# Expert attention scores from rounded and low parts instead of full fp32

## Chip, cores and metric

The kernel runs on one core of a Trainium2 chip. The metric is device time in microseconds (us) of one execution. PE is TensorE, DVE is VectorE, ACT is ScalarE, POOL is GpSimd, PSUM the memory that PE writes.

## What is computed

Three layers follow one another for 4 batches of 576 tokens with 512 features: windowed attention, a gated two-matrix layer, and a mixture of 4 attention experts of width 64 with the best 2 of 4 weighted by a gate. Only the experts matter here:

```python
logits = x @ w_gate
for e in range(E):                      # 4 experts
    q, k, v = x @ wq[e], x @ wk[e], x @ wv[e]          # 576 x 64 each
    scores = scale * (q @ k.transpose(0, 2, 1))
    scores = np.where(causal, -1000000000.0, scores)
    a = np.exp(scores - scores.max(-1, keepdims=True))
    a /= a.sum(-1, keepdims=True) + 1e-09
    ye = a @ v @ wo[e]
    ...                                 # added where e is one of the two chosen
```

## The kernel before

Everything is written out by hand, engine by engine, with semaphores between the engines. The same program runs for the 4 batches; in the first three, the windowed attention of the next batch is worked on beside the dense layer of this one.

**Rounded and low parts.** Most matrix products take operands split in two: `hi` is the value rounded to the type `f32r` (the profile prints it as f32 or fp32r), `lo` is the rest. `pe_passes` (lines 509 to 513) multiplies them in three passes, hi·hi, hi·lo and lo·hi, into one PSUM bank. The scores of the experts do not: `pe_scores` (line 602) multiplies whole fp32 numbers of the tensor `c_kq`, and the profile shows each such matmul as two records.

**The experts' part of a batch** (`pe_experts`, line 692). PE makes 13 projections in the order of the list `PROJECTIONS`: kq 0 to 3 (keys and queries of the first pair of experts, halves of 288 tokens; 0 and 1 are keys, 2 and 3 queries), v 0 to 4 (values and gate logits), kq 4 to 7 (the second pair). They alternate between the two banks of the PSUM tensor `MM`. ACT copies each out (`act_projection`, line 868; the queries are scaled on the way), and its semaphore `mm_out` frees the bank for the projection two further on.

Scores come in 10 tiles, the list `TILES`: for each pair, query tiles of 128 tokens against all keys up to them, so 512, 384, 256 or 128 columns, and the last 64 queries against 576. In this order: 512, 384, 576, 256, 128 columns for the first pair; 512, 576, 384, 256, 128 for the second. The two experts of a pair lie on partitions 0 to 63 and 64 to 127; the matmuls of one use the upper half of PE's rows and those of the other the lower half. For the last tile each expert also has its own half of the output partitions. Tile 0 is scored behind v 4, tile 1 behind kq 6, tile 2 behind the transposes of tile 0; then, in each round of a loop, PE scores tile k+2, transposes the probabilities of tile k and multiplies those of tile k-1 with the values.

Each tile passes through four engines: PE scores (L627 or L621, and the causal mask, L631 or L623), DVE takes the maximum (`dve_c_max`, L1151), ACT the exponential (L840), DVE the sum and its inverse (`dve_c_stat`, L1157 and L1161), POOL scales (L1320), PE transposes (L655), ACT copies (L853, L849, L850), PE multiplies with v (L676). Behind the tiles comes the output projection (`pe_out`, L511 to L513 with `co`), and the next batch.

The wait that guards the tensors is in `pe_scores`: tile 0 waits until kq 2 and 3 are out of PSUM, tile 2 until kq 6 and 7 are, since it also takes both banks of `MM`.

DVE's order in this part is given by `dve_experts`: first half of the gate arithmetic, maxima of tile 0, second half, sums of tile 0, then tile by tile maxima and sums.

Of the kernel before, what the change touches and what calls it, by code (L numbers as in the profile page):

```python
# [27 lines left out]
def build(nc, qk, v, mu, w_k, w_v, w_r, c_v_w, c_k_w, c_q_w, c_o_w, out):  # L28
# [152 lines left out]
    with ctx:  # L181
# [3 lines left out]
        def sem(name):  # L185
            return ctx.enter_context(nc.semaphore(name))
# [45 lines left out]
        def at(name, shape, dt, first):  # L232

            return nc.alloc_sbuf_tensor_at(name, shape, dt, offset=AREA0 + 4 * first)
# [45 lines left out]

        c_kq = at("c_kq", [128, 2 * EP, S], fp32, 2 * K2)
        cv = at("c_v", [TC, NT, NV], fp32, 2 * K2 + 3 * XR)
        assert 2 * K2 + 4 * XR + RING * HALF <= 10112 and NT * NV + S <= XR + RING * HALF
        assert S <= TA * KA
        assert 4 * S <= K2 and 2 * EP * S <= 2 * XR and 4 * S == K2

        c_negmax = sb("c_negmax", [TC, UNITS], fp32)
        c_sum = sb("c_sum", [TC, UNITS], fp32)  # L290
# [51 lines left out]
        pool_passed = sem("pool_passed")  # L342
        gate_step = sem("gate_step")
        gate_exp = sem("gate_exp")
        c_scored = sem("c_scored")
        c_max = sem("c_max")
        c_exp = sem("c_exp")
# [225 lines left out]
        def own(h):  # L573

            return slice(D * h, D * (h + 1))
# [6 lines left out]
        def score_area(k, h):  # L582

            return bank(scores_in(k), h)
# [8 lines left out]
        def prob_tile(u):  # L593

            k, h, _, i = expert_tile(u)
            return cp[k % CP_SETS * 2 + h][:, 0:(i + 1) * TC if i < NT - 1 else S]

        def pe_scores(pe, b, k):
            pair, i = TILES[k]
            m = SIZE[i]  # L600
            if k == 0:

                for n in (2, 3):
                    idx = mm_index("kq", n)
                    pe.wait_ge(mm_out[idx % 2], b * (MMS // 2) + idx // 2 + 2)
            if k == 2:

                for n in range(2):
                    pe.wait_ge(mm_out[n], b * (MMS // 2) + (O0 + 1 - n) // 2 + 1)
            else:  # L610

                before = max(k - 2, 0)
                if k > 0:
                    pe.wait_ge(c_exp, b * UNITS + TILE_UNITS[before].stop)
            if i == NT - 1:

                cut = i * TC
                both = scores_in(k)
                for lo, hi in ((0, cut), (cut, S)):
                    for h in range(2):  # L620
                        nc.tensor.matmul(both[own(h), lo:hi], c_kq[own(h), 2 * pair + 1, cut:S],  # L621
                                         c_kq[own(h), 2 * pair, lo:hi], start=True, stop=hi <= cut)
                last = nc.tensor.matmul(both[:, cut:S], ident2[:, :, :].rearrange("p w n -> p (w n)"),  # L623
                                        causal[0:m, 0:m], start=False, stop=True)
            else:
                for h in range(2):
                    nc.tensor.matmul(score_area(k, h)[:, 0:(i + 1) * TC],  # L627
                                     c_kq[own(h), 2 * pair + 1, i * TC:(i + 1) * TC],
                                     c_kq[own(h), 2 * pair, 0:(i + 1) * TC], start=True, stop=False)
                for h in range(2):  # L630
                    last = nc.tensor.matmul(score_area(k, h)[:, i * TC:(i + 1) * TC], identb[:, :],  # L631
                                            causal[:, :], start=False, stop=True)
            last.then_inc(c_scored, 1)
# [237 lines left out]
        def act_projection(act_, b, what, n):  # L871
            idx = mm_index(what, n)
            act_.wait_ge(mm_full, b * MMS + idx + 1)
            if what == "v":
                nc.scalar.activation(cv[:, n, :], bank(MM, idx % 2)[0:TC, 0:NV], ACT.Copy)\
                    .then_inc(mm_out[idx % 2], 1)
                return
            half = n % 2
            nc.scalar.activation(c_kq[:, n // 2, half * HALF:(half + 1) * HALF], bank(MM, idx % 2)[:, 0:HALF],
                                 ACT.Copy, scale=SCALE if n // 2 % 2 else 1.0).then_inc(mm_out[idx % 2], 1)  # L880

        def act_experts(act_, b):

# [246 lines left out]
        def dve_gates_end(dve, b, step, settled):  # L1130
# [13 lines left out]
            for h in range(2):  # L1144
                one_each = g_exp[0:LAST, NT - 1, :].rearrange("r (p h) -> r p h", h=2)[:, :, h]
                step(nc.vector.tensor_tensor(gates_last[h * LAST:(h + 1) * LAST, :], one_each,
                                             g_sum[0:LAST, NT - 1:NT].broadcast_to([LAST, EP]), ALU.mult))

        def dve_c_max(dve, b, u):
            dve.wait_ge(c_scored, b * PAIR_TILES + expert_tile(u)[0] + 1)  # L1150
            nc.vector.tensor_reduce(c_negmax[:, u:u + 1], scores_of(u), AX.X, ALU.max,  # L1151
                                    negate=True).then_inc(c_max, 1)
# [26 lines left out]
        def dve_experts(dve, b, ahead):  # L1179
            done = [0]  # L1180

            dve_gates(dve, b, done, 0)
            for u in TILE_UNITS[0]:
                dve_c_max(dve, b, u)
            dve_gates(dve, b, done, 1)
            assert done[0] == GATE_STEPS
            for u in TILE_UNITS[0]:
                dve_c_stat(dve, b, u)
            for k in range(1, PAIR_TILES):
                for u in TILE_UNITS[k]:  # L1190
                    dve_c_max(dve, b, u)
                for u in TILE_UNITS[k]:
                    dve_c_stat(dve, b, u)
                if k == Y_SPLIT + 2:
                    dve_y_lo(dve, b, 0)
            if ahead:

                for j in pieces_behind(1, -2)[0:2]:
                    dve_mix(dve, b + 1, j)
            dve_y_lo(dve, b, EP - 1)  # L1200
            if ahead:
                for j in pieces_behind(1, -2)[2:]:
                    dve_mix(dve, b + 1, j)

                for j in pieces_behind(1, -1):
                    dve_mix(dve, b + 1, j)

        def dve_batch(dve, b, ahead):
            for i in range(LAST_STEP):
                dve_dense(dve, b, i)  # L1210
                if ahead:
                    dve_attention(dve, b + 1, i, (SOFT,))
                dve_r(dve, b, i)
                if ahead:
                    dve_attention(dve, b + 1, i, (SCORE, APPLY))
                for j in pieces_behind(b, i):
                    dve_mix(dve, b, j)
                for c in lo_behind(b, i):
                    if DVE_MAKES_LO[c]:
                        dve_chunk(dve, c)  # L1220
            dve_experts(dve, b, ahead)
# [111 lines left out]
        def _(pool):  # L1333
# [46 lines left out]
            for n in range(3):  # L1380
                pool.sem_inc(out_done[n], 1)
            pool.wait_ge(const_step, done)
            nc.gpsimd.affine_select(out=causal[:, :], in_=causal[:, :], compare_op=ALU.is_ge, fill=NEG,
                                    base=0, pattern=[[-1, TC]], channel_multiplier=1).then_inc(const_ready, 1)
            for p, o in FIRST_POOL:
                if p == "mix":
                    pool_mix_lo(pool, 0, o)
                elif p == "lo":
                    pool_chunk(pool, o)
                else:  # L1390
                    pool_step(pool, 0, p, o)
# [61 lines left out]
```

## Time and profile before

| | |
|---|---|
| median of 3 runs | 572.97 us (572.64 to 573.55) |
| the profiled execution: its own time | 571.48 us |
| its span, first to last instruction | 569.7 us |
| PE busy | 544.0 us, 95% of the span |
| DVE, ACT, POOL busy | 339.4, 262.1, 233.4 us |
| scores on the chain that ended last (L627, L621) | 3% and 2% of the span |

Times of an instruction are starts from the beginning of the span and durations; a duration of a matmul includes the time that its data is under way, so matmuls overlap in the rows, and their rate is read from one start to the next. The 1.8 us between span and own time lie before and behind the span.

### The profile page before, as it was taken

The page shows a single profiled execution, that of the slowest core. Times are in us where ns is not written, and L with a number is a line of the kernel's source. Part 1 is how long each engine was busy: PE and PEld are TensorE (multiplying, and loading weights), DVE is VectorE, ACT ScalarE, POOL GpSimd, SP SyncE. Part 2 cuts the span into 40 slices and gives each one's busy share as a digit, 9 for nine tenths or more (in the row PEclk, how much of TensorE's full clock was granted, in tenths as well). Part 3 has the DMA queues.
Part 4 walks back from the last instruction along what each step waited for, and adds up shares of the span by engine and source line. Part 5 has one row for each costly group of instructions (what it writes and reads, how often), then busy time and mean ns, then how long its engine had stood idle before and what let it go on. Part 6 is the DMA issues. An engine that isn't in the chain of part 4 may idle for free.

```text
span 569.7 us, 12200 instructions
## 1 busy us (share of the span) xinstructions
PE 544.0 (95%) x5008; PEld 483.7 (85%) x5008; DVE 339.4 (60%) x696; ACT 262.1 (46%) x656; POOL 233.4 (41%) x285
## 2 busy tenths in 40 slices
PE   6789899999999999999999999999999999999997
PEld 4779799999668989999867989999986799999765
DVE  3998968722577883851458687492156857440561
ACT  3657544223664632423475553332257463322574
POOL 5658655330454642341145364143035555230251
PEclk9889999999999999999999999999999999999999
DMA  8991202210003112111001220100000200000002
GB/s 296 350 319 42 75 13 62 75 33 1 2 1 124 35 44 55 52 46 32 1 2 54 74 75 1 32 1 1 1 2 2 84 2 1 0 1 2 2 1 84
DMA packets 8935, 29.62 MB, mean 52 GB/s; under 512 B 1200, under 2 KB 1200, under 8 KB 8880
## 3 DMA queue, kind: packets, MB, share of 16 engines
q1 hardware_dynamic: 6256, 24.12, 13.2%
q10 hardware_dynamic: 2624, 4.72, 2.6%
q8 instruction: 40, 0.66, 0.5%
q14 instruction: 15, 0.12, 0.1%
HBM read 24.12 MB, written 4.72 MB: 51 GB/s over the span
## 4 chain that ended last, share of the span: by engine, by line
PE 79%; DVE 9%; ACT 5%; POOL 4%; issue 3%; DMA 1%; POOLq 0%; ACTq 0%
PE MM L511 20%; PE MM L513 18%; PE MM L512 18%; PE SC L469 4%; PE OA L676 3%; PE SC L627 3%; PE TR L655 3%; PE OA L500 3%; PE TR L485 2%; ACT c_prob L840 2%; PE MM L621 2%; POOL prob L1263 1%; ACT c_probT L853 1%; DVE row_inv L1016 1%; DVE ring L1073 1%
## 5 line engine op out<-in xcount | busy, mean ns | idle before, releaser
L1292 POOL TENSOR_TENSOR k_lo<-ring,k_hi 128x288 fp32r<-128x288 f32 x64 | 54.4, 851 | 98.1 <-ACT k_hi L821 98.1
L1320 POOL TENSOR_SCALAR c_prob<-c_prob,c_inv,gates 128x512 f32<-128x512 f32 (+3 forms) x64 | 42.1, 666 | 109.9 <-DVE c_inv L1161 109.9
L511 PE MATMUL MM<-k_hi,wv_hi 128*128 128x288 f32 x256 | 76.2, 298 | 4.8 <-DVE ring L1079 2.6
L511 PE MATMUL MM<-act_hi,wk_hi 128*128 128x288 f32 x256 | 77.4, 302 | 0.0
L512 PE MATMUL MM<-k_lo,wv_hi 128*128 128x288 f32 x256 | 75.5, 295 | 0.0
L513 PE MATMUL MM<-k_hi,wv_lo 128*128 128x288 f32 x256 | 75.3, 294 | 0.0
L512 PE MATMUL MM<-act_lo,wk_hi 128*128 128x288 f32 x256 | 75.3, 294 | 0.0
L513 PE MATMUL MM<-act_hi,wk_lo 128*128 128x288 f32 x256 | 75.2, 294 | 0.0
L1093 DVE RECIPROCAL gate_r<-gate_r 128x288 f32<-128x288 f32 x32 | 62.5, 1953 | 1.1
L1073 DVE TENSOR_TENSOR ring<-ring 128x288 f32<-128x288 f32 x64 | 41.3, 653 | 25.6 <-ACT ring L834 25.3
L1048 DVE SCALAR_TENSOR_TENSOR mix<-xT,one_less,mix 128x288 f32<-128x288 f32 x64 | 51.1, 798 | 7.1 <-ACT mix L934 6.0
L511 PEld LDWEIGHTS MM<-k_hi,wv_hi 128*128 128x128 f32 x256 | 48.0, 187 | 5.8 <-DVE ring L1079 3.3
L511 PEld LDWEIGHTS MM<-act_hi,wk_hi 128*128 128x128 f32 x256 | 48.1, 188 | 1.1
L834 ACT ACTIVATE ring<-MM 128x288 f32<-128x288 f32 x64 | 26.2, 409 | 48.8 <-PE MM L513 48.8
L512 PEld LDWEIGHTS MM<-act_lo,wk_hi 128*128 128x128 f32 x256 | 48.2, 188 | 0.0
L513 PEld LDWEIGHTS MM<-k_hi,wv_lo 128*128 128x128 f32 x256 | 48.2, 188 | 0.0
L513 PEld LDWEIGHTS MM<-act_hi,wk_lo 128*128 128x128 f32 x256 | 48.2, 188 | 0.0
L512 PEld LDWEIGHTS MM<-k_lo,wv_hi 128*128 128x128 f32 x256 | 48.1, 188 | 0.0
L511 PE MATMUL MM<-xr_hi,wr_hi 128*128 128x288 f32 x128 | 40.0, 312 | 2.4 <-POOL xr_lo L1280 1.3
L1079 DVE TENSOR_TENSOR ring<-MM,gate_r 128x288 f32<-128x288 f32 x32 | 14.5, 452 | 42.6 <-PE MM L513 42.6
L1292 POOL TENSOR_TENSOR act_lo<-ring,act_hi 128x288 fp32r<-128x288 f32 x32 | 25.5, 805 | 32.4 <-ACT act_hi L821 32.4
L512 PE MATMUL MM<-xr_lo,wr_hi 128*128 128x288 f32 x128 | 38.4, 300 | 0.0
(173 smaller groups left out, 1372.2 us busy)
## 6 DMA issues: line engine op xcount, KB each, us to landing
qkT<-in_qk SPq DMA_DIRECT2D x16, 591.5 KB, 3.8
vn<-in_v SPq DMA_DIRECT2D x16, 432.0 KB, 3.8
out_x<-c_prob ACTq DMA_DIRECT2D x16, 224.0 KB, 2.5
raw_wk_lo<-in_w_k SPq DMA_DIRECT2D x4, 512.0 KB, 17.0
raw_wv_lo<-in_w_v SPq DMA_DIRECT2D x4, 512.0 KB, 19.1
raw_wr_lo<-in_w_r SPq DMA_DIRECT2D x2, 512.0 KB, 8.2
out_x<-c_prob ACTq DMA_DIRECT2D x4, 256.0 KB, 2.8
raw_cv_lo<-in_c_v SPq DMA_DIRECT2D x1, 520.0 KB, 18.0
```

Source lines behind the costliest of these rows:

```text
L469: last = nc.tensor.matmul(tiles[rows, t, :], qT[rows, t * QA:(t + 1) * QA], kT[rows, t * QA:t * QA + KA], start=False, stop=t in (IN_BANK ...
L500: last = nc.tensor.matmul(bank(OA, g)[D * w:D * (w + 1), at_:at_ + hi - lo], vn[0:KA, t, w, :], probT[:, t, w, lo:hi], start=True, stop=True)
L511: nc.tensor.matmul(dst, w2[0], x2[0], start=first, stop=False)
L512: nc.tensor.matmul(dst, w2[0], x2[1], start=False, stop=False)
L513: return nc.tensor.matmul(dst, w2[1], x2[0], start=False, stop=last)
L627: nc.tensor.matmul(score_area(k, h)[:, 0:(i + 1) * TC], c_kq[own(h), 2 * pair + 1, i * TC:(i + 1) * TC], c_kq[own(h), 2 * pair, 0:(i + 1) ...
L834: nc.scalar.activation(ring[:, ITEM[u] % RING, :], src, ACT.Relu)\
L1048: nc.vector.scalar_tensor_tensor(out=slot, in0=xT[:, t, half * HALF:(half + 1) * HALF], scalar=one_less[:, m, t:t + 1], in1=slot, op0=ALU. ...
L1073: nc.vector.tensor_tensor(slot, slot, slot, ALU.mult).then_inc(squared, 1)
L1093: nc.vector.reciprocal(g, g).then_inc(r_step, 1)
L1292: nc.gpsimd.tensor_tensor(lo, ring[:, ITEM[u] % RING, :], hi.bitcast(fp32), ALU.subtract)\
L1320: nc.gpsimd.tensor_scalar(prob_tile(u), prob_tile(u), c_inv[:, u:u + 1], gate, ALU.mult, ALU.mult).then_inc(c_prob, 1)
```

## The change

Keys and queries of the experts are split into a rounded part (`c_kq_hi`, in the place of `c_kq`) and a low part (`c_kq_lo`, new, in the place of an area that is free then). ACT writes the rounded part; DVE then subtracts it from what is still in the PSUM bank (`dve_kq_lo`, one `scalar_tensor_tensor`) and only that frees the bank, so ACT's copy no longer does. Scores of a tile are three passes (`pe_score_passes`), each for both experts. The last 64 queries of a pair are put on the diagonal of a 128x128 tensor `q_last` whose other parts POOL sets to zero once, at the start, and are multiplied over all of PE by `pe_passes`. The projections kq 3 and kq 7, which hold these queries, leave PSUM in three pieces (224 columns, and 64 columns for each expert) on ACT and on DVE.

```diff
+        c_kq_lo = at("c_kq_lo", [128, 2, EP, S], f32r, 0)
...
+        q_last = hl("q_last", [128, EP, TC])
...
+        def kq_parts(n):
+            pair, q_or_k, half = n // 4, n // 2 % 2, n % 2
+            src, first = bank(MM, mm_index("kq", n) % 2)[:, 0:HALF], half * HALF
+            whole = HALF - LAST if (q_or_k, half) == (1, 1) else HALF
+            cols = slice(first, first + whole)
+            parts = [(c_kq[:, n // 2, cols], c_kq_lo[:, q_or_k, pair, cols], src[:, 0:whole])]
+            if whole < HALF:
+                parts += [(*[a[own(h), pair, own(h)] for a in q_last], src[own(h), whole:HALF]) for h in range(2)]
+            return parts
...
+        def pe_score_passes(dst_of, pair, queries, keys, closed):
+            for n, (x, y) in enumerate(((0, 0), (0, 1), (1, 0))):
+                for h in range(2):
+                    nc.tensor.matmul(dst_of(h), c_parts(pair, 1, h, queries)[x], c_parts(pair, 0, h, keys)[y],
+                                     start=n == 0, stop=closed and n == 2)
...
-                    for h in range(2):
-                        nc.tensor.matmul(both[own(h), lo:hi], c_kq[own(h), 2 * pair + 1, cut:S],
-                                         c_kq[own(h), 2 * pair, lo:hi], start=True, stop=hi <= cut)
+                    pe_passes(both[:, lo:hi], [a[:, pair, :] for a in q_last],
+                              [c_kq[:, 2 * pair, lo:hi], c_kq_lo[:, 0, pair, lo:hi]], True, hi <= cut)
...
-            nc.scalar.activation(c_kq[:, n // 2, half * HALF:(half + 1) * HALF], bank(MM, idx % 2)[:, 0:HALF],
-                                 ACT.Copy, scale=SCALE if n // 2 % 2 else 1.0).then_inc(mm_out[idx % 2], 1)
+            for dst, _, src in kq_parts(n):
+                last = nc.scalar.activation(dst, src, ACT.Copy, scale=scale)
+            last.then_inc(c_kq_hi_out, 1)
...
+        def dve_kq_lo(dve, b, n):
+            dve.wait_ge(c_kq_hi_out, b * 4 * EP + n + 1)
...
+            for hi, lo, src in kq_parts(n):
+                last = nc.vector.scalar_tensor_tensor(out=lo, in0=src, scalar=SCALE if n // 2 % 2 else 1.0,
+                                                      in1=hi.bitcast(fp32), op0=ALU.mult, op1=ALU.subtract)
+            last.then_inc(mm_out[mm_index("kq", n) % 2], 1)
...
+            for n in range(1, 4):
+                dve_kq_lo(dve, b, n)
...
+            for t in q_last:
+                nc.gpsimd.memset(t[:, :, :].bitcast(fp32), 0.0).then_inc(q_last_zeroed, 1)
```

**DVE behind kq 4.** The low parts of kq 0 (in `dve_batch`, ahead of copies of the next batch's attention) and of kq 1 to 3 come before this place. Before, behind the maxima of tile 0 (L1151) came the second half of the gates:

```order
L1151 TENSOR_REDUCE c_negmax<-SC 128x1 x2
L1133 SCALAR_TENSOR_TENSOR g_exp<-g_dif,g_exp 128x20
L1136 TENSOR_REDUCE g_sum<-g_exp 128x5
L1138 TENSOR_SCALAR g_sum<-g_sum 128x5
L1140 RECIPROCAL g_sum<-g_sum 128x5
L1142 TENSOR_TENSOR gates<-g_exp,g_sum 128x20
L1146 TENSOR_TENSOR gates_last<-g_exp,g_sum 64x2 x2
```

With the change:

```order
L1191 TENSOR_REDUCE c_negmax<-SC 128x1 x2
L1185 SCALAR_TENSOR_TENSOR c_kq_lo<-MM,c_kq_hi 128x288
L1163 SCALAR_TENSOR_TENSOR g_exp<-g_dif,g_exp 128x20
L1166 TENSOR_REDUCE g_sum<-g_exp 128x5
L1168 TENSOR_SCALAR g_sum<-g_sum 128x5
L1170 RECIPROCAL g_sum<-g_sum 128x5
L1172 TENSOR_TENSOR gates<-g_exp,g_sum 128x20
L1176 TENSOR_TENSOR gates_last<-g_exp,g_sum 64x2 x2
L1185 SCALAR_TENSOR_TENSOR c_kq_lo<-MM,c_kq_hi 128x288
```

The low part of kq 4 stands behind the maxima, that of kq 5 behind the gates.

**DVE around the second tile.** Before, the maxima of tile 1 (the L1151 row on `SC`) stood behind the sums of tile 0 and were followed by the sums of tile 1 and the maximum of tile 2:

```order
L1157 TENSOR_SCALAR c_inv<-c_sum 128x1
L1161 RECIPROCAL c_inv<-c_inv 128x1
L1151 TENSOR_REDUCE c_negmax<-SC 128x1 x2
L1157 TENSOR_SCALAR c_inv<-c_sum 128x1
L1161 RECIPROCAL c_inv<-c_inv 128x1
L1157 TENSOR_SCALAR c_inv<-c_sum 128x1
L1161 RECIPROCAL c_inv<-c_inv 128x1
L1151 TENSOR_REDUCE c_negmax<-MM 128x1
```

With the change:

```order
L1197 TENSOR_SCALAR c_inv<-c_sum 128x1
L1201 RECIPROCAL c_inv<-c_inv 128x1
L1185 SCALAR_TENSOR_TENSOR c_kq_lo<-MM,c_kq_hi 128x288
L1191 TENSOR_REDUCE c_negmax<-SC 128x1 x2
L1185 SCALAR_TENSOR_TENSOR c_kq_lo<-MM,c_kq_hi 128x224
L1185 SCALAR_TENSOR_TENSOR q_last_lo<-MM,q_last_hi 64x64 x2
L1197 TENSOR_SCALAR c_inv<-c_sum 128x1
L1201 RECIPROCAL c_inv<-c_inv 128x1
L1197 TENSOR_SCALAR c_inv<-c_sum 128x1
L1201 RECIPROCAL c_inv<-c_inv 128x1
L1191 TENSOR_REDUCE c_negmax<-MM 128x1
```

The low part of kq 6 stands ahead of the maxima of tile 1, the three pieces of kq 7 stand behind them and ahead of the sums of tile 1.

**PE, tile 2**, the last 64 queries of the first pair, before (each row names matmuls of the program, of which a whole fp32 one is two in the profile):

```order
L621 MATMUL MM<-c_kq 64x512 x2
L621 MATMUL MM<-c_kq 64x64 x2
L623 MATMUL MM<-causal,ident 128x64
L627 MATMUL SC<-c_kq 128x256 x2
L631 MATMUL SC<-causal,identb 128x128 x2
```

With the change:

```order
L518 MATMUL MM<-c_kq_hi,q_last_hi 128x512
L519 MATMUL MM<-c_kq_lo,q_last_hi 128x512
L520 MATMUL MM<-c_kq_hi,q_last_lo 128x512
L518 MATMUL MM<-c_kq_hi,q_last_hi 128x64
L519 MATMUL MM<-c_kq_lo,q_last_hi 128x64
L520 MATMUL MM<-c_kq_hi,q_last_lo 128x64
L652 MATMUL MM<-causal,ident 128x64
L625 MATMUL SC<-c_kq_hi 128x256 x2
L625 MATMUL SC<-c_kq_lo,c_kq_hi 128x256 x2
L625 MATMUL SC<-c_kq_hi,c_kq_lo 128x256 x2
L658 MATMUL SC<-causal,identb 128x128 x2
```

The last tile is six matmuls over all of PE; an ordinary tile (the 256 columns of tile 3 here) is three pairs.

## Rows read from the trace of the kernel before

**Rows 1.** The page: span, busy time of the engines, granted clock of PE.

```profile
span 569.7 us, 12200 instructions
...
PE 544.0 (95%) x5008; PEld 483.7 (85%) x5008; DVE 339.4 (60%) x696; ACT 262.1 (46%) x656; POOL 233.4 (41%) x285
...
PEclk9889999999999999999999999999999999999999
```

**Rows 2.** Timeline of PE: start us, us, engine, line, operation, out<-in, shapes, count.

```profile
136.21 1.13 PE L627 MATMUL SC<-c_kq 64*128 64x512 f32 x4
137.27 0.28 PE L631 MATMUL SC<-causal,identb 128*128 128x128 bf16 x2
...
142.35 0.92 PE L627 MATMUL SC<-c_kq 64*128 64x384 f32 x4
143.20 0.29 PE L631 MATMUL SC<-causal,identb 128*128 128x128 bf16 x2
...
144.97 1.04 PE L655 MATMUL TR<-identf,c_prob 128*128 128x128 f32 x8
145.93 1.19 PE L621 MATMUL MM<-c_kq 64*64 64x512 f32 x8
147.06 0.20 PE L623 MATMUL MM<-causal,ident 64*128 64x64 bf16 x1
147.06 0.71 PE L627 MATMUL SC<-c_kq 64*128 64x256 f32 x4
147.70 0.29 PE L631 MATMUL SC<-causal,identb 128*128 128x128 bf16 x2
```

**Rows 3.** The same timeline: last matmul of kq 3, first of v 0, first of v 1.

```profile
128.81 0.30 PE L513 MATMUL MM<-act_hi,cq_lo 128*128 128x288 f32 x1
128.95 0.28 PE L511 MATMUL MM<-cv_hi,act_hi 128*128 128x260 f32 x1
...
130.38 0.28 PE L511 MATMUL MM<-cv_hi,act_hi 128*128 128x260 f32 x1
```

**Rows 4.** Matmuls and weight loads on c_kq from 136.5 to 136.76 us: duration ns min/median/max.

```profile
L627 PE MATMUL SC<-c_kq x4: 589/641/693, 136.2 to 136.7; 64*128 64x512 f32 x4
L627 PEld LDWEIGHTS SC<-c_kq x1: 186/186/186, 136.3 to 136.3; 64*128 64x128 f32 x1
```

**Rows 5.** Timeline of ACT; in brackets the idle time before, and what ended it.

```profile
145.17 0.41 ACT L879 ACTIVATE c_kq<-MM 128x288 f32<-128x288 f32 x1 [2.29 <-PE MM L513]
...
151.19 0.60 ACT L849 ACTIVATE c_probT<-TR 128x512 f32<-128x512 f32 x1 [0.51 <-PE TR L655]
151.69 0.26 ACT L850 ACTIVATE c_probT<-TR 64x128 f32<-64x128 f32 x1
```

**Rows 6.** Timeline of DVE, the same columns.

```profile
120.29 0.46 DVE L1079 TENSOR_TENSOR ring<-MM,gate_r 128x288 f32<-128x288 f32 x1 [2.74 <-PE MM L513]
...
165.54 0.52 DVE L1048 SCALAR_TENSOR_TENSOR mix<-xT,one_less,mix 128x288 f32<-128x288 f32 x1
...
168.31 0.76 DVE L1175 TENSOR_TENSOR k_hi<-OA,k_hi 128x576 fp32r<-128x576 f32 x1 [0.17 <-ACT k_hi L869]
```

**Rows 7.** The chain that ended last, first batch: start us, us, what.

```profile
149.51 0.83 POOL c_prob L1320
150.39 0.77 PE TR L655 x5
...
160.37 0.55 ACT y_raw L859
...
165.65 0.75 POOL c_prob L1320
```

**Rows 8.** Timeline of POOL: the start of the program, and tile 0's second scaling.

```profile
7.25 0.29 POOL L1383 TENSOR_SCALAR_AFFINE_SELECT causal<-causal 128x128 bf16<-128x128 bf16 x1
8.97 2.35 POOL L1329 TENSOR_TENSOR wr_lo<-raw_wr_lo,wr_hi 128x1024 fp32r<-128x1024 f32 x1 [1.43 <-ACT wr_hi L970]
...
142.52 0.77 POOL L1320 TENSOR_SCALAR c_prob<-c_prob,c_inv,gates 128x512 f32<-128x512 f32 x1 [0.47 <-DVE c_inv L1161]
```

More of the change, by code:

```diff
@@ L279, in build @@
         y_raw = at("y_raw", [128, S], fp32, EP * S)
-        c_kq = at("c_kq", [128, 2 * EP, S], fp32, 2 * K2)
+        c_kq = at("c_kq_hi", [128, 2 * EP, S], f32r, 2 * K2)
+        c_kq_lo = at("c_kq_lo", [128, 2, EP, S], f32r, 0)
         cv = at("c_v", [TC, NT, NV], fp32, 2 * K2 + 3 * XR)
@@ L344, in build @@
         gate_exp = sem("gate_exp")
+        c_kq_hi_out = sem("c_kq_hi_out")
+        q_last_zeroed = sem("q_last_zeroed")
         c_scored = sem("c_scored")
@@ L596, in prob_tile, with c_parts @@
             return cp[k % CP_SETS * 2 + h][:, 0:(i + 1) * TC if i < NT - 1 else S]
+        def kq_parts(n):
[7 more added lines that the diff above has]
+            return parts
+        def c_parts(pair, q_or_k, h, cols):
+            return c_kq[own(h), 2 * pair + q_or_k, cols], c_kq_lo[own(h), q_or_k, pair, cols]
+        def pe_score_passes(dst_of, pair, queries, keys, closed):
[3 more added lines that the diff above has]
+                                     start=n == 0, stop=closed and n == 2)
         def pe_scores(pe, b, k):
@@ L625, in pe_scores @@
             else:
[L626 to L629, printed above, removed]
+                pe_score_passes(lambda h: score_area(k, h)[:, 0:(i + 1) * TC], pair,
+                                slice(i * TC, (i + 1) * TC), slice(0, (i + 1) * TC), False)
                 for h in range(2):
@@ L877, in act_projection @@
                 return
-            half = n % 2
-            nc.scalar.activation(c_kq[:, n // 2, half * HALF:(half + 1) * HALF], bank(MM, idx % 2)[:, 0:HALF],
-                                 ACT.Copy, scale=SCALE if n // 2 % 2 else 1.0).then_inc(mm_out[idx % 2], 1)
+            scale = SCALE if n // 2 % 2 else 1.0
+            if n % 4 == 3:
+                act_.wait_ge(q_last_zeroed, 2)
+            for dst, _, src in kq_parts(n):
+                last = nc.scalar.activation(dst, src, ACT.Copy, scale=scale)
+            last.then_inc(c_kq_hi_out, 1)
         def act_experts(act_, b):
@@ L1147, in dve_gates_end @@
                                              g_sum[0:LAST, NT - 1:NT].broadcast_to([LAST, EP]), ALU.mult))
+        def dve_kq_lo(dve, b, n):
+            dve.wait_ge(c_kq_hi_out, b * 4 * EP + n + 1)
+            if n % 4 == 3:
+                dve.wait_ge(q_last_zeroed, 2)
+            for hi, lo, src in kq_parts(n):
+                last = nc.vector.scalar_tensor_tensor(out=lo, in0=src, scalar=SCALE if n // 2 % 2 else 1.0,
+                                                      in1=hi.bitcast(fp32), op0=ALU.mult, op1=ALU.subtract)
+            last.then_inc(mm_out[mm_index("kq", n) % 2], 1)
         def dve_c_max(dve, b, u):
@@ L1184, in dve_experts @@
                 dve_c_max(dve, b, u)
+            dve_kq_lo(dve, b, 4)
             dve_gates(dve, b, done, 1)
             assert done[0] == GATE_STEPS
+            dve_kq_lo(dve, b, 5)
             for u in TILE_UNITS[0]:
                 dve_c_stat(dve, b, u)
+            dve_kq_lo(dve, b, 6)
+            for u in TILE_UNITS[1]:
+                dve_c_max(dve, b, u)
+            dve_kq_lo(dve, b, 7)
             for k in range(1, PAIR_TILES):
                 for u in TILE_UNITS[k]:
-                    dve_c_max(dve, b, u)
+                    if k > 1:
+                        dve_c_max(dve, b, u)
                 for u in TILE_UNITS[k]:
@@ L1213, in dve_batch @@
                 dve_r(dve, b, i)
+                if i == LAST_STEP - 1:
+                    dve_kq_lo(dve, b, 0)
                 if ahead:
@@ L1384, in _ @@
                                     base=0, pattern=[[-1, TC]], channel_multiplier=1).then_inc(const_ready, 1)
+            pool.wait_ge(const_ready, 2)
+            for t in q_last:
+                nc.gpsimd.memset(t[:, :, :].bitcast(fp32), 0.0).then_inc(q_last_zeroed, 1)
             for p, o in FIRST_POOL:
```

## The prediction, as put on record

> **What bounds the kernel now.** I read the page first. PE is busy for 544.0 of 569.7 us and its granted clock is 9 tenths or more in all but two of 40 slices, both in the first three [rows 1]; at this clock, 2.4 GHz, a pass over N columns streams for N/2.4 ns. So only what shortens PE's own queue, or a wait in it, can help; DVE at 60%, ACT at 46% and POOL at 41% have room on average. The change lies in one stretch of each batch, some 46 us long, from kq 0 to the output projection. In its first part, to 145 us in the first batch, PE's timeline has no gap: a projection follows a projection, with the scores of tiles 0 and 1 between them. In its second part, the loop over tiles, the chain of waits alternates: PE, then the softmax of a tile on DVE, ACT and POOL, then PE [rows 7]. What is saved in the first part is saved only if nothing new is waited for at the seam, at tile 2.
>
> **Scores, what a tile costs.** From its first matmul to the first of its causal mask, a tile of 512, 384 or 256 columns takes 1.06, 0.85, 0.64 us [rows 2]. That is 4N/2.4 (0.85, 0.64, 0.43) and 0.21 more each time: four passes, with the two experts side by side (each pair starts as one, two records at 136.2, two at 136.7 [rows 4]). By the same form 128 columns take 0.42. The first pair lasts 693 ns and the second 589 [rows 4], so 0.10 of the 0.21 is the wait for the first weights; the other 0.11 lies before the mask, which uses other rows of PE.
>
> The changed tile has three passes. A pass costs N/2.4 and a gap: v 0, 12 matmuls of 260 columns, takes 1.43 us [rows 3], so 0.119 each, 0.108 streaming and 0.011 gap. No row shows a rounded matmul under 260 columns. The nearest are eight transposes with 128, 0.96 us from their first to the next matmul [rows 2]; without the 0.10 for the next one's weights 0.11 each, twice the 0.053 of streaming. I take 0.11 as the least of any pass, and keep 0.053 and 0.213 (four times the streaming, as a whole fp32 matmul) as bounds for 128 columns. With 0.21 kept:
> - 512: 3 x 0.224 + 0.21 = 0.88, saves 0.18
> - 384: 3 x 0.171 + 0.21 = 0.72, saves 0.13
> - 256: 3 x 0.118 + 0.21 = 0.56, saves 0.08
> - 128: 3 x 0.11 + 0.21 = 0.54, costs 0.12
>
> The last 64 queries took 1.13 us, 145.93 to 147.06 [rows 2]. Now: three passes of 512 over all of PE, 0.67; three of 64 columns, two at 0.11 and the last only its 0.03 of streaming; and 0.10 before the mask, which uses half the rows. That is 1.02, saving 0.11. Its bounds are 0.91 (nothing before the mask) and 1.13.
>
> **The low part, what it costs.** ACT's copy of 288 columns takes 0.41 [rows 5], as before. DVE's low part reads PSUM and SBUF and writes SBUF: the nearest row is L1079 with 0.46, with 576 columns 0.76 [rows 6], so 0.16 and 1.04 ns a column. The same operation from SBUF alone took 0.52 [rows 6], the upper end. For six of the eight projections of a batch, 0.41 + 0.46 and about 0.25 of signalling make 1.1 us, inside the 1.57 (12 x 0.131) of the projection that runs in the other bank: cost nothing. DVE is idle there (2.74 us before L1079 [rows 6]). On ACT the fetch is not longer. The low parts of kq 4 and 5 also stand ahead of the sums of tile 0 and move them by up to 2 x 0.46; POOL ended tile 0 at 143.29 [rows 8] and PE turned it at 144.97 [rows 2], 1.68 later: covered. If that cover went, PE would wait at the turn of tile 0, and that is not near.
>
> kq 3 and kq 7 leave in three pieces. ACT: L849 and L850 show that a following piece starts 0.50 after one of 0.60, so 0.10 overlap, and that 128 columns last 0.26 [rows 5]; 224 and twice 64 columns come to 0.26 + 0.13 + 0.22 = 0.61. DVE, with 0.08 overlap: 0.31 + 0.15 + 0.23 = 0.69. Bounds: 0.50 and 0.55 if pieces overlap more, 0.88 and 0.95 if they don't at all.
>
> **Where it is waited for.** Two places.
> - v 1 needs the bank of kq 3. kq 3's last matmul gives way at 128.95 [rows 3]; ACT starts 0.20 later (144.97 to 145.17 at kq 7 [rows 2, 5]), ends at 129.76, DVE from 129.80 to 130.49, PE at 130.54 instead of 130.38 [rows 3]: costs 0.16.
> - Tile 2 needs kq 7. Tiles 0 and 1 save 0.18 + 0.13, so kq 7 ends at 144.97 + 0.16 - 0.31 = 144.82. PE then turns tile 0 until 145.78. ACT works from 145.02 to 145.63, DVE from 145.67 to 146.36, PE at 146.41, where it started at 145.93 before [rows 2]: 0.48 later, with 0.63 of new idle time. The maxima of tile 1 stand ahead of this low part on DVE, but the mask of tile 1 starts at 143.20 before [rows 2] and some 0.15 earlier now, and two maxima over 384 columns, about 0.5 us each by the same 1.04 ns a column, end by 144.5: they cost it nothing. Behind it wait only the sums of tile 1, which wait for ACT anyway.
>
> **The sum, one batch.** Tile 2 starts 0.48 late and is scored 0.37 late. Its softmax releases PE's turn of tile 2 (POOL to 150.34, PE at 150.39 [rows 7]), so 0.37 late; tiles 3 and 4 lie in front of that wait and count for nothing. Then tile 5 takes off 0.18, tile 6 0.11, tile 7 0.13: 0.05 early. From there ACT is the chain up to y_raw [rows 7], started by PE, so still 0.05 early; tile 8 lies in front of it. Tile 9's extra 0.12 is taken up where PE waits for POOL's last tile [rows 7]. The zeros of `q_last` fall into POOL's 1.43 us of idle time before 8.97 [rows 8] (the mask of 128x128 beside them took 0.29), and cost nothing. Four batches: -0.2 us against the profiled execution's 571.48, so 571.3; the runs' median lies 1.5 higher, and by the same difference I forecast 572.8. PE loses 0.7 us of work a batch and waits for nearly all of it.
>
> **A rule against it.** The rows show that weights are loaded under a running pass of the same rows: a load begins at 136.3, 0.4 us before the second pair starts, and that pair is 0.10 shorter than the first [rows 4]. The Trainium skill, "TensorE: Matmul & The Clock Gate", Part 3, says that LDWEIGHTS overlaps running matmuls only when the row group differs. By that rule this trace disagrees for fp32; what it would give for three passes is rival E.
>
> **Rivals**, against 572.97, where 0.2% or 1.15 us is about what can be told from no change:
> - **A, as summed**, 0.37: 572.8.
> - **B, faster**, 0.33: pieces overlap more (0.50 and 0.55) and the last tiles take 0.91. The wait at v 1 goes (0.16), tile 2's shrinks by 0.25, two last tiles give 0.22: 0.68 a batch with the 0.05, so 570.3. For it: L850 starts 0.10 before L849 ends, with other operands and in the same order [rows 5]. Against: no row shows a piece of 64 columns read from PSUM.
> - **C, slower, the wait for kq 7's low part decides**, 0.10: pieces overlap not at all, both waits grow by 0.53, 1.0 a batch with the 0.05: 577.0, and 575 half way. With ACT's and DVE's pieces together 0.02 over my 1.30 us the gain is gone, with 0.17 over it the change is slower by 0.2%.
> - **D, narrow passes are dear**, 0.12: 3 x 0.224 for 128 columns instead of 3 x 0.11, 0.34 more in tiles 4 and 9; less the slack before the turn of tile 2 (0.2) 0.5 a batch: 574.8. No row speaks against it.
> - **E, loads don't hide**, 0.05: 0.10 for each of two more passes in tiles 0, 1, 5, 7, and 0.3 in each last tile: 1.4 a batch, 578.6. The rule above is this rival; the rows speak against it.
> - **F, the experts' passes don't run side by side** as rounded ones, so that three passes are six, 0.03: 0.67 in tiles 0 and 5, 0.51 in 1 and 7, 2.4 a batch: 582.4. The pairs of rows 4 speak against it.
>
> **The numbers.** A is the likeliest: 572.8. Faster is B, 0.33; within 0.2% is A, 0.37; slower C to F, 0.30. The range reaches down past B for the lower bound of the gap (nothing instead of 0.011 for some 15 passes a batch, 0.2 us, four times), 569.5, and up past D and half of C, 575.8. That leaves out the rest of C, E and F, 0.13, and some below. A's own range is 571.8 to 574.0.
>
> **What would show it.** Pairs of passes 0.22 apart at 512 columns, 0.11 at 128; 0.88 from tile 0's first matmul to its mask; last tiles at 1.02. ACT's pieces 0.61 and DVE's 0.69 in all. An idle time of PE of about 0.6 before tile 2, released by DVE, and 0.16 before v 1, in each batch; projections 0 to 2 and 4 to 6 without a wait. The turn of tile 2 still released by POOL, 0.37 later than before. Wrong if tile 2 starts as early as 145.8 (B) or after 146.9 (C), if a pass of 128 columns takes 0.2 (D), or if rounded passes of the two experts don't start together (F).

## The result: slower by 0.45%, and the profile after

The changed kernel takes 574.96 us (median of 8 runs, 574.14 to 575.36), the kernel before beside it 572.81 us. The ratio is 1.0045, 95% interval 1.0034 to 1.0057: slower by 1.9 to 3.3 us. The forecast was 572.8 us, no change.

The page of the changed kernel, in the lines of [rows 1]:

```profile
span 573.2 us, 12378 instructions
...
PE 542.6 (95%) x5056; PEld 491.1 (86%) x5056; DVE 355.4 (62%) x744; ACT 264.3 (46%) x672; POOL 233.4 (41%) x287
...
PEclk9989999999999999999999999999999999999999
```

PE's busy time fell by 1.4 us and the span grew by 3.5: PE got less to do and waits more. Its list of waits names the new one (what PE waited for, us in total, times, the longest); the y_raw row was 2.9 us in 4 waits before, and the row with `q_last_lo` did not exist:

```profile
PE OA L703 <- ACT y_raw L886: 3.2, 4, 0.8
PE MM L518 <- DVE q_last_lo L1185: 2.8, 4, 0.7
```

PE's timeline of the first batch (start us, duration us), for [rows 2]: tiles 0 and 1, the turn of tile 0, tiles 2 and 3.

```profile
137.11 0.50 PE L625 MATMUL SC<-c_kq_hi 64*128 64x512 f32 x2
137.44 0.40 PE L625 MATMUL SC<-c_kq_lo,c_kq_hi 64*128 64x512 f32 x2
137.68 0.40 PE L625 MATMUL SC<-c_kq_hi,c_kq_lo 64*128 64x512 f32 x2
138.01 0.29 PE L658 MATMUL SC<-causal,identb 128*128 128x128 bf16 x2
...
143.09 0.45 PE L625 MATMUL SC<-c_kq_hi 64*128 64x384 f32 x2
...
143.82 0.28 PE L658 MATMUL SC<-causal,identb 128*128 128x128 bf16 x2
...
145.58 1.03 PE L682 MATMUL TR<-identf,c_prob 128*128 128x128 f32 x8
147.31 0.50 PE L518 MATMUL MM<-c_kq_hi,q_last_hi 128*128 128x512 f32 x1 [0.70 <-DVE q_last_lo L1185]
147.65 0.40 PE L519 MATMUL MM<-c_kq_lo,q_last_hi 128*128 128x512 f32 x1
147.88 0.39 PE L520 MATMUL MM<-c_kq_hi,q_last_lo 128*128 128x512 f32 x1
148.11 0.19 PE L518 MATMUL MM<-c_kq_hi,q_last_hi 128*128 128x64 f32 x1
...
148.46 0.20 PE L652 MATMUL MM<-causal,ident 64*128 64x64 bf16 x1
```

Read start to start: tile 0 takes 0.90 us and not 1.06, tile 1 0.73 and not 0.85. From the first transpose of tile 0 to tile 2 there are 1.73 us where [rows 2] have 0.96. Tile 2 itself takes 1.15, 1.13 before. The same view at v 0 and v 1, for [rows 3]:

```profile
129.32 0.30 PE L520 MATMUL MM<-act_hi,cq_lo 128*128 128x288 f32 x1
...
131.19 0.39 PE L518 MATMUL MM<-cv_hi,act_hi 128*128 128x260 f32 x1
131.41 0.28 PE L519 MATMUL MM<-cv_lo,act_hi 128*128 128x260 f32 x1
```

v 0 began at 129.46, so v 1, 1.43 us of matmuls later, was due at 130.89 and waits 0.30; and its first matmul takes 0.22 to the next start where the others take 0.12. The reason stands in the timelines of ACT and DVE, kq 3 and then kq 7 (for [rows 5]; in brackets the idle time before, and what ended it):

```profile
129.66 0.36 ACT L909 ACTIVATE c_kq_hi<-MM 128x224 fp32r<-128x224 f32 x1 [1.18 <-PE MM L520]
129.91 0.43 ACT L909 ACTIVATE q_last_hi<-MM 64x64 fp32r<-64x64 f32 x2
...
145.78 0.36 ACT L909 ACTIVATE c_kq_hi<-MM 128x224 fp32r<-128x224 f32 x1 [2.17 <-PE MM L520]
```

```profile
130.38 0.39 DVE L1185 SCALAR_TENSOR_TENSOR c_kq_lo<-MM,c_kq_hi 128x224 fp32r<-128x224 f32 x1 [1.41 <-ACT q_last_hi L909]
130.69 0.45 DVE L1185 SCALAR_TENSOR_TENSOR q_last_lo<-MM,q_last_hi 64x64 fp32r<-64x64 f32 x2
...
146.50 0.39 DVE L1185 SCALAR_TENSOR_TENSOR c_kq_lo<-MM,c_kq_hi 128x224 fp32r<-128x224 f32 x1 [1.33 <-ACT q_last_hi L909]
146.81 0.45 DVE L1185 SCALAR_TENSOR_TENSOR q_last_lo<-MM,q_last_hi 64x64 fp32r<-64x64 f32 x2
```

ACT's three pieces take 0.68 us (129.66 to 130.34), DVE's 0.76 (130.38 to 131.14), and DVE starts only when ACT has ended. PE starts 0.05 later. At kq 7 it is the same, with DVE idle 1.33 us before it.

The batches of both kernels repeat this to 0.06 us, but for the part behind tile 2 in the last one, which is 0.4 us shorter, before as after. The table gives, for every kernel of this study (the last row from the second of its two profiles), the start-to-start times of the first batch in PE's timeline: v 0 to the turn of tile 0 (A), on to tile 2 (B), on to tile 2's mask (C), on to the output projection (D), and the sum.

| kernel | A | B | C | D | sum | against before |
|---|---|---|---|---|---|---|
| before | 16.02 | 0.96 | 1.13 | 20.45 | 38.56 | |
| the change | 16.12 | 1.73 | 1.15 | 20.31 | 39.31 | +0.75 |
| no low parts | 15.73 | 0.94 | 1.15 | 20.52 | 38.34 | -0.22 |
| before + low parts, three pieces | 16.42 | 1.73 | 1.12 | 20.44 | 39.71 | +1.15 |
| before + low parts, one piece | 16.01 | 1.16 | 1.12 | 20.43 | 38.72 | +0.16 |
| the change, undivided copies | 15.70 | 1.15 | 1.15 | 20.34 | 38.34 | -0.22 |
| that, last tiles in fp32 | 15.70 | 1.15 | 1.13 | 20.18 | 38.16 | -0.40 |
| the change, low part of kq 7 first | 16.11 | 1.73 | 1.15 | 21.11 | 40.10 | +1.54 |
| undivided copies, tile 6 in fp32 | 15.70 | 1.16 | 1.14 | 20.16 | 38.16 | -0.40 |

Between the output projection and the next batch's kq 0 nothing changed (91.23 and 91.26 us). So the change costs 4 x 0.75 = 3.0 us, inside the interval of the comparison. Of the rest of the 3.5 us between the two spans, 0.5 lies ahead of the first batch (kq 0 starts at 121.50 and 120.99); in the profiles of this study, but for one of 1,775 us (below), that start lies anywhere from 120.85 to 123.45, so nothing ties the 0.5 to the change.

### The profile page after: what moved, and what is told of

The parts are those of the page before. It is cut to its first block, busy times and chain, and to the rows that moved or that the text cites. A ratio compares the mean times of both kernels' runs of the same rounds, so it can differ in the third digit from the quotient of the medians.

```text
span 573.2 us, 12378 instructions
## 1 busy us (share of the span) xinstructions
PE 542.6 (95%) x5056; PEld 491.1 (86%) x5056; DVE 355.4 (62%) x744; ACT 264.3 (46%) x672; POOL 233.4 (41%) x287
## 4 chain that ended last, share of the span: by engine, by line
PE 76%; DVE 11%; ACT 5%; POOL 4%; issue 3%; DMA 1%; POOLq 0%; ACTq 0%
PE MM L518 20%; PE MM L520 18%; PE MM L519 18%; PE SC L476 4%; PE OA L703 3%; PE SC L625 3%; PE OA L507 3%; PE TR L682 2%; PE TR L492 2%; ACT c_prob L867 2%; DVE row_inv L1046 2%; POOL prob L1314 1%; DVE mix L1078 1%; ACT c_probT L880 1%; DVE ring L1103 1%
```

## Experiments

The theories after the result. **W**: the two waits for the three-piece copies cost all of it. **P**: the loss is in PE's new passes themselves, above all in those of the last tiles. The first four kernels were compared with the same 29 runs of the kernel before (median 572.22 us), the next two with 17 (572.66), the last version and the repeat of the change with 12 (572.82).

### No low parts

The low parts are left out: DVE makes none, ACT's copy frees the bank as before, and each pass takes the rounded part in its place.

```diff
-            return c_kq[own(h), 2 * pair + q_or_k, cols], c_kq_lo[own(h), q_or_k, pair, cols]
+            return [c_kq[own(h), 2 * pair + q_or_k, cols]] * 2
...
-            last.then_inc(c_kq_hi_out, 1)
+            last.then_inc(mm_out[mm_index("kq", n) % 2], 1)
```

> The changed kernel without the low parts: VectorE computes none, ScalarE's copy frees the bank again, and the three passes all read the rounded parts (that part of the computation is left out). TensorE's instructions are those of the change. Theory W (the loss of 2.1 us is waiting for the low parts): v 1 doesn't wait, tile 2 starts 0.96 us after the turn of tile 0, tiles 0 and 1 save 0.28, tile 5 0.15, tile 7 0.13, the last tiles together cost 0.1, so about 0.45 a batch less than the kernel before: 571.0 us. Theory P (TensorE's own new passes cost what is lost, above all the last tiles over the whole array): no gain over the kernel before, 573 to 575 us.

Measured: 572.09 us, ratio 0.9996 [0.998, 1.0011]. In total time that is no difference from the kernel before; the trace tells more. B is back at 0.94. Against the change the waits give back 0.97 a batch (39.31 to 38.34), more than the whole loss, so W holds and P does not: taken together, the passes alone lose nothing. But without any wait they gain 0.22 a batch, half of W's 0.45, so they save less than I summed. A gains 0.29 by tiles 0 and 1; D loses 0.07 although tiles 5 and 7 are cheaper. One reason is in PE's row behind tile 3:

```profile
148.88 1.19 PE L682 MATMUL TR<-identf,c_prob 128*128 128x128 f32 x6
```

The six transposes of tile 1 take 0.82 us in the kernels before and after and 1.19 here: PE is early and has to wait for tile 1's probabilities inside them. POOL's scalings of tile 1 end at 149.46, and the second three transposes start at 149.52. So tile 2's mask comes 0.29 earlier, but the turn of tile 2 stands 3.55 us behind it (151.62 less 148.07) and not 3.33 as before: 0.22 is lost there. From that turn to the output projection it is 16.97 and not 17.12. Once the waits are gone, tile 1's softmax is the next bound.

### The kernel before with the low parts alone

Two kernels score in fp32 as before, but DVE makes all low parts, in the change's order, and frees the banks. In the first, kq 3 and kq 7 leave in three pieces as in the change, in the second whole. Nobody reads the low parts.

```diff
+            parts = [(c_kq[:, n // 2, cols], c_kq_lo[:, q_or_k, pair, cols], src[:, 0:whole])]
+            if whole < HALF:
+                rest = slice(first + whole, first + HALF)
+                parts += [(c_kq[own(h), n // 2, rest], c_kq_lo[own(h), q_or_k, pair, rest],
+                           src[own(h), whole:HALF]) for h in range(2)]
```

Three pieces:

> The kernel before, its fp32 scores untouched, with the low parts computed on VectorE and freeing the banks as in the change, kq 3 and 7 in three pieces on both engines; nothing reads them. Theory W: v 1 starts 0.40 late, tile 2 another 0.77 late and with 0.10 for its first weights, 1.27 a batch: 577.9 us. Theory P: at most 1 us over the kernel before.

Measured: 577.28 us, ratio 1.0088 [1.0066, 1.011]; theory W, with 1.15 us a batch and not 1.27, since its 0.10 for the first weights of tile 2 did not come (C is 1.12). The wait before tile 2 is that of the change, in total, count and length:

```profile
PE MM L636 <- DVE c_kq_lo L1169: 2.8, 4, 0.7
```

One piece (`whole` is `HALF` everywhere):

> The same with kq 3 and 7 in one piece of 288 columns on both engines. Theory W with the pieces as the dear part: v 1 doesn't wait (0.20 + 0.41 + 0.04 + 0.46 + 0.05 = 1.16 us against the 1.43 of v 0), tile 2 waits 0.20 and 0.10 for its weights: 0.3 a batch, 574.0 us. If it is the low part as such and not its pieces: near the run with three pieces, 577 us or more.

Measured: 573.34 us, ratio 1.0017 [1.0005, 1.003]. v 1 doesn't wait (A 16.01), and B is 1.16, 0.20 more than before. So the low parts themselves cost 0.16 us a batch; cutting them in three costs 0.99 more (39.71 less 38.72): 0.41 at v 1 and 0.57 at tile 2. This is the main cost of the change, measured with nothing else in it. The passes then give 0.40 back (39.71 to 39.31), and 0.16 + 0.99 - 0.40 is the change's 0.75.

### The change with undivided copies

kq 3 and kq 7 leave whole; GpSimd fills `q_last` from the last 64 columns, by a product with a tensor of ones and zeros, for the first pair ahead of its scalings and for the second ahead of the scaling of tile 2.

```diff
-            whole = HALF - LAST if (q_or_k, half) == (1, 1) else HALF
+            whole = HALF
...
+                nc.gpsimd.tensor_tensor(dst[:, pair, :].rearrange("p (w n) -> p w n", w=2),
+                                        src.bitcast(fp32).unsqueeze(1).broadcast_to([128, 2, LAST]),
+                                        diagonal[:, :, :], ALU.mult).then_inc(q_last_in, 1)
```

> The changed kernel with kq 3 and 7 leaving PSUM in one piece of 288 columns on ScalarE and VectorE; GpSimd builds the diagonal tensor of the last queries afterwards, from SBUF, by a product with a constant of ones and zeros (two operations a pair). Theory W: v 1 doesn't wait, tile 2 starts 0.2 us after the turn of tile 0 ends instead of 0.77, about 0.9 a batch less than the change, 0.16 less than the kernel before: 571.4 to 572.3 us. Theory P: within 1 us of the change, 574 to 575 us.

Measured: 571.27 us, ratio 0.9978 [0.9965, 0.9992]: slightly faster than the kernel before, and by the table 0.97 us a batch better than the change; theory W. DVE's row for kq 3 is

```profile
132.06 0.46 DVE L1184 SCALAR_TENSOR_TENSOR c_kq_lo<-MM,c_kq_hi 128x288 fp32r<-128x288 f32 x1 [1.13 <-ACT c_kq_hi L910]
```

behind 0.41 us of ACT: 0.87 for both engines where the pieces take 1.44.

### The last tiles in fp32 again

In that kernel the two last tiles are scored as before, one fp32 matmul per half of the rows, from the rounded parts alone.

```diff
-                    pe_passes(both[:, lo:hi], [a[:, pair, :] for a in q_last],
-                              [c_kq[:, 2 * pair, lo:hi], c_kq_lo[:, 0, pair, lo:hi]], True, hi <= cut)
+                    for h in range(2):
+                        nc.tensor.matmul(both[own(h), lo:hi], c_kq[own(h), 2 * pair + 1, cut:S].bitcast(fp32),
+                                         c_kq[own(h), 2 * pair, lo:hi].bitcast(fp32), start=True, stop=hi <= cut)
```

> The kernel with undivided copies and low parts (571.27 us), with the two last tiles of each batch (tiles 2 and 6) scored as the kernel before scores them: an fp32 matmul for each half of the rows, first the 512 columns, then the 64. Both halves read the rounded parts alone, so the low parts are left out of these two tiles' products; all copies, low parts, their waits and GpSimd's fills stay. It tells what the three whole-array passes of a last tile cost in their place. Theory W (my forecast's term: a last tile costs 0.11 us less in three passes than in fp32, wherever it stands): taking them away costs 0.11 us at tile 2 and 0.11 at tile 6, 0.22 a batch, so 572.1 us, and tile 6 with the multiply behind it stays at 2.03 us or grows. Theory Q (what the two traces show: before, the fp32 matmuls of tile 6 in one half of the rows run while the 64-column multiplies ahead of them are still going, and passes over the whole array wait for these to end): tile 6 with its multiply goes back from about 2.03 us to about 1.85, tile 2 from 1.15 to 1.13, first multiply of the result from tile 2's mask back by 0.15 to 0.2 us, so 570.5 us.

Measured: 570.46 us, ratio 0.9964 [0.9947, 0.9982]. Theory W's 572.1 us would be a ratio of 0.9998 and is excluded. Whether anything was gained over the kernel above the totals don't tell, since the two intervals overlap; the trace does, with 38.16 for 38.34: theory Q. Tile 6 in this kernel, PE's timeline:

```profile
155.11 0.89 PE L707 MATMUL OA<-c_probT,c_v 128*64 128x64 f32 x18
155.75 0.64 PE L654 MATMUL MM<-c_kq_hi 64*64 64x512 f32 x1
155.83 0.23 PE L707 MATMUL OA<-c_probT,c_v 64*64 64x64 f32 x2
155.89 1.13 PE L654 MATMUL MM<-c_kq_hi 64*64 64x512 f32 x7
156.96 0.20 PE L656 MATMUL MM<-causal,ident 64*128 64x64 bf16 x1
```

and in the change:

```profile
154.84 0.95 PE L703 MATMUL OA<-c_probT,c_v 128*64 128x64 f32 x20
155.72 0.50 PE L518 MATMUL MM<-c_kq_hi,q_last_hi 128*128 128x512 f32 x1
...
156.87 0.20 PE L652 MATMUL MM<-causal,ident 64*128 64x64 bf16 x1
```

In fp32 the first scores start at 155.75, ahead of the last two multiplies at 155.83: from the multiplies' first to the mask 1.85 us. The passes over the whole array start behind all 20 multiplies, 0.88 after the first of them instead of 0.64, and it is 2.03. The trace of before has 1.85 too (153.61 to 155.46), with the same order:

```profile
153.61 0.89 PE L676 MATMUL OA<-c_probT,c_v 128*64 128x64 f32 x18
154.24 0.64 PE L621 MATMUL MM<-c_kq 64*64 64x512 f32 x1
...
155.46 0.20 PE L623 MATMUL MM<-causal,ident 64*128 64x64 bf16 x1
```

### The low part of kq 7 ahead of the maxima of tile 1

One part of the change undone.

```diff
-            for u in TILE_UNITS[1]:
-                dve_c_max(dve, b, u)
             dve_kq_lo(dve, b, 7)
+            for u in TILE_UNITS[1]:
+                dve_c_max(dve, b, u)
```

> One part of the change undone: on VectorE the low part of kq 7 stands ahead of the maxima of tile 1 and not behind them. Everything else is as in the change. If the place of the maxima matters as the change has it (VectorE fills its wait for ScalarE's copy of kq 7 with them; in the trace it idles 1.33 us behind them before this low part), putting them behind the low part frees PE's bank not a moment sooner, since the low part waits for ScalarE: tile 2 starts at the same time, and the statistics of tile 1 and what hangs on them (its exponentials, its turn) come about 1 us later. Theory H (that delay is hidden: PE's turn of tile 1's probabilities comes after tile 2's scores and waits for GpSimd): 575.0 us, the same as the change. Theory L (tile 1's turn is what PE waits for after tile 2): the turn comes up to 1 us later in each batch, up to 579 us. Between them the part of 1 us that is not covered decides; I expect 0.3 to 0.6 us a batch, 576.2 to 577.4.

Measured: 578.87 us, ratio 1.0109 [1.0078, 1.014], 3.9 us above the change's first median (3.7 by the ratios), more than I expected. Tile 2 starts where it did (B 1.73), and behind it PE meets a new wait, one in each batch:

```profile
PE SC L625 <- ACT c_prob L867: 2.0, 4, 0.5
```

Tile 3 needs the bank of tile 1, which is free when ACT has taken the exponentials, and these start 2.30 us behind the first transpose of tile 0, in the change 0.91. With the turn of tile 1 behind it D grows by 0.80. So theory L: as long as DVE makes the low part of kq 7, having the maxima ahead of it is worth 0.8 us a batch, and this part of the change should stay. In the last batch it was more, and for another reason. Busy time by stretches of 2 us, with the granted clock in the column behind POOL:

```profile
543.00:545.00 2.00, 1.40 (x9) 1.12 (x9) 1.45 (x6) 1.34 (x5) 0.08 (x1) 1.00 0.00 0
545.00:547.00 2.00, 2.00 (x14) 1.46 (x14) 1.06 (x4) 1.90 (x5) 1.23 (x2) 0.67 0.00 0
547.00:549.00 2.00, 2.00 (x17) 1.58 (x16) 1.44 (x7) 1.59 (x6) 1.06 (x2) 0.50 0.00 0
```

Behind the two idle times of 0.70 and 0.51 us the granted clock fell to 0.50, that is 1.2 GHz, for about 3 us, and the 16 multiplies of tile 0 took 1.98 us instead of 1.09. D of this batch is 21.97, in the change 19.91.

### A version from these results

Undivided copies, tile 2 in three passes, tile 6 in fp32, from the sum of rounded and low part that GpSimd makes.

```diff
+            nc.gpsimd.tensor_tensor(dst, c_kq[:, 2 + q_or_k, cols].bitcast(fp32),
+                                    c_kq_lo[:, q_or_k, 1, cols].bitcast(fp32), ALU.add).then_inc(q_last_in, 1)
...
+                            nc.tensor.matmul(both[own(h), lo:hi], kq_sum[own(h), S:S + LAST],
+                                             kq_sum[own(h), lo:hi], start=True, stop=hi <= cut)
```

> A version made from what the runs before showed: undivided copies and low parts (571.27 us), tile 2 in three passes, and tile 6 alone in fp32 as the kernel before has it, from keys and queries that GpSimd puts together again (rounded plus low part: one addition of 576 columns between its scalings of tiles 0 and 1, where it idles 2.8 us, one of 64 columns ahead of its scaling of tile 2, in place of the two products that filled q_last for this pair). Theory Q (the fp32 matmuls of one half of the rows overlap the 64-column multiplies ahead of them): tile 6 with its multiply 1.85 us and not 2.03, 0.18 a batch, 0.7 in all: 570.5 us. Theory S (GpSimd's additions come late: its scalings of tiles 1 and 2 move back and PE's turns wait for them): turn of tile 1 and later up to 0.5 us a batch later, up to 573 us. I expect 570.5.

Measured: 570.70 us (median of 7), ratio 0.9958 [0.9942, 0.9973] from six of them, so 2.4 us faster than the kernel before, and as forecast. The seventh, the profiled one, took 1,775 us (below), so the kernel ran once more:

> The same kernel as the run before it, for a trace: its profiled execution took 1,775 us, with the matmuls of 288 columns at 0.74 us each where every other profile of this program has 0.29, and the other six took 569.9 to 570.7; it tells nothing of the kernel. Theory Q: tile 6 with its multiply 1.85 us, 38.16 us from the first matmul of v to the first of the output projection, GpSimd's addition of 576 columns about 1 us inside its idle 2.8 us, its scaling of tile 2 no later after tile 2's scores than in the version with undivided copies. Theory S: that scaling, and PE's turn of tile 2 behind it, later by up to 0.5 us.

This single execution took 571.89 us (kq 0 of the first batch at 122.88, a late start). Theory Q: the sum is 38.16, tile 6 with its multiply 1.85, and GpSimd:

```profile
144.01 1.52 POOL L1400 TENSOR_SCALAR c_prob<-c_prob,c_inv,gates 128x512 f32<-128x512 f32 x2 [11.11 <-DVE c_inv L1206]
145.50 1.43 POOL L1367 TENSOR_TENSOR kq_sum<-c_kq_hi,c_kq_lo 128x576 f32<-128x576 f32 x1
148.31 1.30 POOL L1400 TENSOR_SCALAR c_prob<-c_prob,c_inv,gates 128x384 f32<-128x384 f32 x2 [1.38 <-DVE c_inv L1206]
```

The addition took 1.43 us and not my "about 1", and 1.38 of idle time are left behind it.

### The change once more

> The changed kernel as it is, once more, beside the version above and further runs of the kernel before on one chip: 575.0 us, ratio to the kernel before 1.0045; its four batches should each take 0.75 us more from the first matmul of v to the first of the output projection, as in its first profile, and the start-up ahead of the first batch should differ from that profile by up to some tenths of a us either way, since it did so between the profiles so far.

Measured: 575.45 us, ratio 1.005 [1.0033, 1.0068]: the same loss again. The first batch took 39.36, +0.80 against before, and the next ones 39.37, 39.32 and, in the last, 38.90 (before 38.13 there). kq 0 of the first batch started at 122.02.

## Why the prediction was wrong

574.96 us lies inside the range, but I forecast no change, and the change is slower, clear of the noise. My sum said -0.05 us a batch, the trace says +0.75. Where PE waits and for whom was right. What failed are three terms of the sum: the three pieces of a copy (1.30 forecast, 1.44 measured, paid twice), the first weights (nothing forecast; 0.10 at v 1, 0.13 in tile 2), and the overlap at tile 6, which I left out (0.11 to be saved, 0.18 lost). The steps, in the order of the prediction:

- **Tiles over one expert per half of the rows**: right. 0.88, 0.72, 0.56 and 0.54 were forecast for 512, 384, 256 and 128 columns; 0.90, 0.73, 0.57 and 0.48 came. Pairs start together, 0.24 apart at 512 columns and 0.12 at 128: rivals D and F did not happen. Rival E did not either: 512 columns stream for 0.213 us, and the next pass over the same rows starts 0.23 to 0.24 behind, which leaves no room for a load of 0.18 to 0.19. The profile has the load for the pass of 137.68 start at 137.44, with the pass before it. The Trainium skill's sentence behind rival E, that weight loads overlap running matmuls only where the row group differs ("TensorE: Matmul & The Clock Gate", Part 3), disagrees with this trace for rounded operands too, while the other case that the same part names, a load into the background weight buffer, would fit it.
- **The last tiles**: wrong. I put 1.02 where 1.15 came. The step was "three passes of 512 over all of PE, 0.67": they take 0.80 (147.31 to 148.11), since the first has 0.34 to the next start and the others 0.23. I had kept the 0.10 of the first weights for the ordinary tiles and left it out here. That is 0.13 at tile 2. At tile 6 it is 0.29: "tile 6 0.11" was to be saved, and 0.18 was lost, because the fp32 matmuls had overlapped the multiply ahead of them, which the timeline of before shows at 154.24 and which I never costed. The kernels with this tile in fp32 show it: 0.18 a batch back.
- **The pieces**: the mechanism was right, the size too small. ACT 0.68 and not 0.61, DVE 0.76 and not 0.69, so 1.44 and not 1.30, inside my bounds. The piece of 224 columns came as forecast (0.25 and 0.31 to the next start); the two of 64 columns take 0.43 and 0.45 where I had 0.35 and 0.38. I had let each piece overlap the next, by 0.10 on ACT and 0.08 on DVE. ACT's first two do (129.91 against an end at 130.02), but its two of 64, of 0.21 each, take 0.43 together: no overlap. It counts at both places: 0.14 at v 1, 0.14 at tile 2.
- **v 1**: forecast 0.16, came 0.40. Besides the 0.14, the first matmul behind a wait takes 0.10 us more to the next start. Its weight load starts together with it (both at 131.18 to 131.19), where in PE's queue without a gap a load starts one matmul ahead of its own. I priced the wait without that.
- **Tile 2**: forecast 0.48 late, came 0.87 (A and B together); against the turn of tile 0, 0.63 forecast and 0.77 measured. It was released by DVE as said. **The place of the maxima**: they "cost it nothing", right; what the other order would cost, 0.8 us a batch, I had not priced and did not need.
- **POOL's zeros**: 0.31 us each, at 7.58 and 7.83 us, with 1.09 us still idle behind them: nothing, as said. **The turn of tile 2** was released by POOL, as said.

By the columns of the table, forecast and measured changes are -0.15 and +0.10 for A, +0.63 and +0.77 for B, -0.11 and +0.02 for C, -0.42 and -0.14 for D: 0.25, 0.14, 0.13 and 0.28 off, 0.80 in all. A is off by the longer pieces (0.14) and the first weights (0.10), B by the longer pieces, C by the first weights of the last tile, D by tile 6 (0.29). Rival C, which had 0.10 of the chance, is right in its mechanism and covers a third of the miss: it said that 0.02 us over my 1.30 for the pieces takes the gain and that 0.17 makes it slower by 0.2%; 0.14 came, which by its own sum gives +0.23 us a batch and 573.9 us. The other 0.52 a batch, the first weights and tile 6, stood in no rival, so that the time came out near C's "575 half way" is luck. A case whose point of decision lies 0.02 us from the sum, on a term whose bounds were 1.05 and 1.83, deserved far more.

Without any wait the change would have gained 0.22 us a batch and not 0.36, which the tiles alone give (0.16, 0.12, 0.15 and 0.13 for tiles 0, 1, 5 and 7, less 0.18 and 0.02 for tiles 6 and 2), since PE then meets the softmax of tile 1. With undivided copies the same 0.22 is left for another reason: B keeps 0.19 of the wait for DVE. What stays open is whether kq 7's low part could be made without lengthening the time of the bank; it wasn't tried.

## What to carry over

When a PSUM bank has to be read by two engines in turn, the second read adds its whole length to the time that the bank is held, and pieces add a fixed cost each on both engines: find where PE needs that bank next before cutting a copy, and let an idle engine rearrange afterwards. Price a new wait of PE with the weight load that it uncovers, and a matmul's new form with what the old form overlapped, not by its passes alone. Where the sum is near zero, a term with wide bounds decides the sign and deserves much of the chance, and a term left at nothing needs a row that shows it.

## Hardware behaviour that was not expected

- Small pieces: ACT's copy of 288 columns takes 0.41 us, the same data as 224 columns on 128 partitions and 64 columns on each half 0.68; DVE's subtraction 0.46 and 0.76. ACT's second piece starts 0.10 before the first has ended, its third only when the second has.
- Score matmuls with 64 rows by 64 columns of PE start while the last multiplies ahead of them in the program are still starting (155.75 ahead of 155.83), and matmuls over all of PE do not. These multiplies read partitions 0 to 63, and of the two experts' scores one reads 64 to 127; that it is this one that starts early is likely, but the profile doesn't name the rows.
- In one batch of one kernel the granted clock fell from 1.00 to 0.50 behind two idle times of 0.5 to 0.7 us, and the three batches before, with the same idle times, show nothing of it (D 21.10 to 21.13 in each). Why only one did stays open.
- One execution of the last version took 1,775 us, where its others took 569.9 to 571.9. Its page has a mean granted clock of 1.00, the other engines busy for about as long as always (ACT 265.5 us, DVE 343.8), and the matmuls of 288 columns more than twice as long as on every other page, here beside the page of the next execution of the same kernel:

```profile
L521 PE MATMUL MM<-act_hi,wk_hi 128*128 128x288 f32 x256 | 190.6, 745 | 0.0
```

```profile
L521 PE MATMUL MM<-act_hi,wk_hi 128*128 128x288 f32 x256 | 77.4, 302 | 0.0
```

Nothing in the kernel explains it, and nothing here does; it was not seen again.
